# The widest exponential between two upper parts, and weight jobs in quarters

## The reference

```python
scores = np.where(mask, q @ k.T / np.sqrt(64), -1e9)
attn = softmax(scores)                 # row max taken off, sum + 1e-9
x = (attn @ v)                         # to (2304, 512)
h = x @ w_in                           # 512 x 2048
x = (h * np.clip(h + 3, 0, 6) / 6) @ w_out          # first layer
h = x @ w_in2
out = (h * np.tanh(np.log1p(np.exp(h)))) @ w_out2   # second layer
```

## Time and profile before

| what | value |
|---|---|
| median of 3 runs | 994.08 us (991.94 to 994.55) |
| the profiled execution | 992.28 us, with a span of 990.5 us |
| TensorE matmuls busy | 962.7 us (97%) |
| VectorE busy | 758.6 us (77%) |
| ScalarE busy | 644.6 us (65%) |
| GpSimd busy | 446.9 us (45%) |
| mean granted clock | 0.998 of full speed |

### The profile page before, as it was taken

One profiled execution on the slowest core, in us unless ns is written; L12 is line 12 of the kernel. 1 busy time (PEld: TensorE's weight loads), 2 busy tenths in 40 slices (PEclk: granted clock), 3 DMA queues, 4 the chain that ended last, 5 costly groups with the idle time before them and its releaser, 6 DMA issues.

```text
span 990.5 us, 17992 instructions
## 1 busy us (share of the span) xinstructions
PE 962.7 (97%) x6132; PEld 859.8 (87%) x6132; DVE 758.6 (77%) x1443; ACT 644.6 (65%) x1429; POOL 446.9 (45%) x412
## 2 busy tenths in 40 slices
PE   6999899999999999999999999999999999999998
PEld 5888898999888898898889888899889898898896
DVE  5888898978686766769798786876877877777654
ACT  6888788856454554544446556777777777776663
POOL 6776899867765576969676680000000000000000
PEclk9999999999999999999999999999999999999999
DMA  7778667754789978587967545646645645465255
GB/s 163 212 188 253 169 175 203 189 154 145 236 274 326 301 264 285 182 288 273 330 226 259 220 149 177 238 151 219 237 162 211 234 177 196 170 231 201 90 189 194
DMA packets 81914, 211.49 MB, mean 214 GB/s; under 512 B 12320, under 2 KB 19104, under 8 KB 81824
## 3 DMA queue, kind: packets, MB, share of 16 engines
q1 hardware_dynamic: 81744, 210.06, 65.1%
q10 hardware_dynamic: 80, 0.29, 0.1%
HBM read 170.39 MB, written 39.92 MB: 212 GB/s over the span
## 4 chain that ended last, share of the span: by engine, by line
PE 77%; DVE 6%; ACT 2%; DMA 2%; issue 1%; SPq 1%; ACTq 0%; DVEq 0%
PE psum L962 35%; PE psum L845 11%; PE psum L847 11%; PE psum L846 11%; PE psum L795 3%; PE psum L774 3%; PE psum L752 2%; PE psum L754 1%; DVE ebuf L1514 1%; PE psum L750 1%; DVE glo L1520 1%; DVE xlo L1449 1%; DMA ext_d<-ext_made 1%; DMA o_d<-staged 1%; DVE ext_made L1420 1%
## 5 line engine op out<-in xcount | busy, mean ns | idle before, releaser
L962 PE MATMUL psum<-ghi,osplit 128*128 128x512 f32 (+1 forms) x640 | 215.9, 371 | 0.4 <-POOL osplit L1767 0.4
L845 PE MATMUL psum<-xhi,whi 128*128 128x256 f32 (+1 forms) x640 | 187.4, 293 | 2.2 <-ACT snap L1163 2.0
L847 PE MATMUL psum<-xhi,wlo 128*128 128x256 f32 (+1 forms) x640 | 186.8, 292 | 0.0
L846 PE MATMUL psum<-xlo,whi 128*128 128x256 f32 (+1 forms) x640 | 186.6, 292 | 0.0
L962 PE MATMUL psum<-osplit,ghi 128*128 128x512 f32 x576 | 180.9, 395 | 1.1 <-DVE glo L1520 0.9
L1520 DVE SCALAR_TENSOR_TENSOR glo<-ebuf,ghi 128x512 fp32r<-128x512 f32 x144 | 124.0, 861 | 24.8 <-ACT ghi L1211 16.8
L845 PEld LDWEIGHTS psum<-xhi,whi 128*128 128x128 f32 x640 | 120.8, 189 | 15.2 <-ACT snap L1163 3.6
L1767 POOL TENSOR_TENSOR osplit<-oraw,osplit 128x512 fp32r<-128x512 f32 x80 | 115.2, 1442 | 38.4 <-ACT osplit L1130 34.2
L962 PEld LDWEIGHTS psum<-ghi,osplit 128*128 128x128 f32 x640 | 117.9, 189 | 16.4 <-issue 0.6
L1211 ACT ACTIVATE ghi<-ebuf 128x512 fp32r<-128x512 f32 x144 | 90.2, 627 | 62.9 <-DVE ebuf L1514 34.4
L846 PEld LDWEIGHTS psum<-xlo,whi 128*128 128x128 f32 x640 | 120.8, 189 | 10.7
(11 more groups left out here) (113 smaller groups left out, 2250.8 us busy)
## 6 DMA issues: line engine op xcount, KB each, us to landing
ext<-ext_d SPq DMA_DIRECT2D x56, 768.0 KB, 4.3
osplit<-o_d SPq DMA_DIRECT2D x80, 512.0 KB, 5.6
oraw<-in_w_out SPq DMA_DIRECT2D x80, 256.0 KB, 5.6
qkin<-in_qk SPq DMA_DIRECT2D x63, 288.0 KB, 4.4
wraw<-in_w_in SPq DMA_DIRECT2D x32, 512.0 KB, 5.6
ext_d<-ext_made SPq DMA_DIRECT2D x32, 384.0 KB, 5.5
attn_t<-ostage SPq DMA_DIRECT2D x64, 144.0 KB, 3.2
o_d<-staged SPq DMA_DIRECT2D x32, 256.0 KB, 5.2
```

What stands on the lines that cost most here:

```text
L845: pe.matmul(dst, hi, xh, start=(start and cc == 0), stop=False, skip_group_check=True)
L846: pe.matmul(dst, hi, xl, start=False, stop=False, skip_group_check=True)
L847: last = pe.matmul(dst, lo, xh, start=False, stop=(stop and cc == 1), skip_group_check=True)
L962: last = pe.matmul(bank(Y_BANK + c, n), stat, mov, start=(first and m == 0), stop=(final and m == 2), skip_group_check=True)
```

## The change

ScalarE makes the widest exponential between upper parts 0 and 1 instead of behind both. The split of x (steps 21 to 23) moves from the end of ScalarE's step to behind the exponential of tile 1. The first four weight jobs are cut in four pieces of 256 columns, one piece a step: pieces of job m are in ScalarE's steps 1+4m to 4+4m behind the exponential of tile 1, and in VectorE's steps 2+4m to 5+4m behind the second copy. The mixing of job m is in VectorE's step 4m, at the same place, ahead of the piece. The loads of weights move from steps 0, 1, 4, 7, 10, 13 to -1, 3, 7, 11, 15, 19. The counts that others wait for follow from a table, `SPLIT`.

```diff
-EARLY_JOBS = {3: 0, 6: 1, 9: 2, 12: 3}
+QUARTERS, QUARTER_JOBS = 4, 4
+FIRST_QUARTER = [1 + QUARTERS * m for m in range(QUARTER_JOBS)]
-EARLY_LOADS = {0: 0, 1: 1, 4: 2, 7: 3, 10: 4, 13: 5}
+EARLY_LOADS = {-1: 0, 3: 1, 7: 2, 11: 3, 15: 4, 19: 5}
...
+def quarter_at(h):
+
+    for m in range(QUARTER_JOBS):
+        if 0 <= h - FIRST_QUARTER[m] < QUARTERS:
+            return ((m, h - FIRST_QUARTER[m]),)
+    return ()
...
+SPLIT = [sum(QUARTERS if k < QUARTER_JOBS else 1 for k in range(m)) for m in range(len(JOBS) + 1)]
...
                 if m >= 2:
-                    sp.wait_ge(w_lo, m - 1)
+                    sp.wait_ge(w_lo, SPLIT[m - 1])
...
             def attention_step(n):
                 if in_use(n):
                     split_probs_hi(n, 0)
+                    exps(n, 4)
                     split_probs_hi(n, 1)
-                    exps(n, 4)
                 if in_use(n + 3) and n < -1:
                     split_q_hi(n + 3)
                 if in_use(n + 1):
                     exps(n + 1, 0)
-                if in_use(n + 1):
                     exps(n + 1, 1)
+                for m, k in quarter_at(n):
+                    split_quarter_hi(m, k)
+                if n in EARLY_X_HI:
+                    split_x_hi(0, 0, EARLY_X_HI.index(n))
                 if in_use(n):
                     split_probs_hi(n, 3)
...
-                if n in EARLY_X_HI:
-                    split_x_hi(0, 0, EARLY_X_HI.index(n))
-                if n in EARLY_JOBS:
-                    split_res_hi(EARLY_JOBS[n])
+
+            def split_quarter_hi(m, k):
+                act.wait_ge(w_mixed, MIXED[m + 1])
+                cols = slice(k * A_COLS, (k + 1) * A_COLS)
+                nc.scalar.activation(whi[m][:, cols], wraw[m % 2][:, cols], ACT.Copy).then_inc(w_hi, 1)
...
                     copy_o(n, 1)
                     if n % HEADS == HEADS - 1:
                         invert_sums(n // HEADS)
+                if n + 1 in FIRST_QUARTER:
+                    mix_w(FIRST_QUARTER.index(n + 1))
+                for m, k in quarter_at(n - 1):
+                    split_quarter_lo(m, k)
                 if in_use(n + 2):
                     row_max(n + 2, 2)
...
-                if n + 1 in EARLY_JOBS:
-                    mix_w(EARLY_JOBS[n + 1])
-                if n in EARLY_JOBS:
-                    split_res_lo(EARLY_JOBS[n])
...
+            def split_quarter_lo(m, k):
+                dve.wait_ge(w_hi, SPLIT[m] + k + 1)
+                cols = slice(k * A_COLS, (k + 1) * A_COLS)
+                nc.vector.tensor_tensor(wlo[m][:, cols], wraw[m % 2][:, cols], whi[m][:, cols].bitcast(F32),
+                                        ALU.subtract).then_inc(w_lo, 1)
```

More of the change, by code:

```diff
@@ L542, in store_ext_hi @@
                 layer, p = JOBS[m][0:2]
-                sp.wait_ge(w_hi, m + 1)
+                sp.wait_ge(w_hi, SPLIT[m + 1])
                 sp.dma_start(ext_d[layer, p, :, 0:EXT], ext_made[:, 0:EXT].bitcast(F32)).then_inc(ext_hi_stored, 16)
@@ L547, in store_ext_lo @@
                 layer, p = JOBS[m][0:2]
-                sp.wait_ge(w_lo, m + 1)
+                sp.wait_ge(w_lo, SPLIT[m + 1])
                 sp.dma_start(ext_d[layer, p, :, EXT:], ext_made[:, EXT:].bitcast(F32)).then_inc(ext_lo_stored, 16)
@@ L570, in load_ahead @@
                 elif t in (8, 9):
-                    sp.wait_ge(w_lo, 2 * PAIRS - 1 + t % 2)
+                    sp.wait_ge(w_lo, SPLIT[2 * PAIRS - 1 + t % 2])
                 if t >= 2 and t not in (8, 9):
@@ L627, in load_x @@
                         return
-                    sp.wait_ge(w_lo, len(JOBS))
+                    sp.wait_ge(w_lo, SPLIT[len(JOBS)])
                     for i in range(2):
@@ L836, in weights_ready @@
                 if BLOCK_OF[g] % NBL == 0:
-                    pe.wait_ge(w_lo, (3 * PAIRS if layer_of(g) else 0) + p + 1)
+                    pe.wait_ge(w_lo, SPLIT[(3 * PAIRS if layer_of(g) else 0) + p + 1])
             def accumulate(dst, a_hi, a_lo, g, b, n, start, stop):
@@ L1410, in split_res_lo @@
                 p = JOBS[m][1]
-                dve.wait_ge(w_hi, m + 1)
+                dve.wait_ge(w_hi, SPLIT[m + 1])
                 nc.vector.tensor_tensor(wlo[p][:, :], wraw[m % 2][:, :], whi[p][:, :].bitcast(F32), ALU.subtract
                                         ).then_inc(w_lo, 1)
+            def split_quarter_lo(m, k):
[3 more added lines that the diff above has]
+                                        ALU.subtract).then_inc(w_lo, 1)
             def split_ext_lo(m):
                 layer, p = JOBS[m][0:2]
-                dve.wait_ge(w_hi, m + 1)
+                dve.wait_ge(w_hi, SPLIT[m + 1])
                 if layer * PAIRS + p > 0:
```

## The result

The changed kernel took 1009.23 us, median of four runs (1005.41 to 1011.83), beside 993.27 for the kernel before (991.94 to 994.55). The ratio is 1.0158, with a 95% interval of 1.0117 to 1.0199: slower, by 16 us. The forecast was 1002.5, with a range of 994 to 1011. The profiled execution took 1011.1 us, the slower side of its runs, with a span of 1009.3; that of before had 990.5. So the two traces lie 18.8 us apart, where the medians lie 16 apart.

What follows compares the result with a forecast made beforehand. TensorE, busy 97% of 990.5 us, was taken as the bound. Terms: -11.5 - 1.5 + 12.3 + 4.5 + 5.5 = +9.3, giving 1002.5 us as the middle of two bases; range 994 to 1011.

Steps and rivals of the forecast that it cites:

- The late loads: VectorE's four mixings wait for weights that land after the copy; 12.3 us in sum, bounds 0 and 25.
- job 3: Fourth weight job: load issued behind two x chunks, VectorE waits 2.7 us, 3.2 with mix and quarter less slack.
- c: End of VectorE's copy of the second half of a head's attention result; 22.35 us in a clean head.
- The clock: TensorE's granted clock falls to 0.50 behind three of four waits, 1.5 us each; 4.5 us, bounds 0 and 6.
- The old jobs: The four weight jobs' old cost in the heads, x loads among them, vanishes whole; -11.5 us.
- The quarters: VectorE's quarter subtractions collide with GpSimd's q subtraction; thirteen outside mixing heads, ten at 0.5, three at 0.15; 5.5 us.
- My sign of being wrong: Wrong if VectorE shows no wait for the weights, or quarter heads stay at 5.8 to 5.9 us.
- VectorE's gap of 0.19 us: Idle gap on VectorE after its second copy, counted within about 0.2 us of slack in a clean head.
- The exponential: ScalarE's 576-column exponential one upper part earlier helps only where TensorE waits for it; costed at nothing.
- The x heads: Three heads carrying a split of x, which nearly fits ScalarE's idle time, return to 5.80 us; -1.5 us.

Runs made afterwards that it cites:

- early_loads: The changed kernel with its four weight loads moved to steps -2, 1, 5 and 9 (from -1, 3, 7, 11); 992.95 us, ratio 1.0001.
- x_one_later: exp_first with GpSimd's adding and scaling of x one step later and the splits of x in every second step; 987.00 us, ratio 0.9947.
- exp_first: The kernel before with only the widest exponential between upper parts 0 and 1 and the split of x behind tile 1's exponential; 990.97 us, ratio 0.9977.
- early_loads_lo_last: early_loads with VectorE's quarter subtraction moved from ahead of tile 2's row maximum to behind tile 3's; 991.86 us, ratio 0.9997.
- hi_quarters_mix_early: hi_quarters_lo_whole with the mixing one step earlier and the loads at -3, 1, 5, 9; 989.35 us, ratio 0.9975.
- hi_quarters_lo_whole: x_one_later with ScalarE's upper parts of four jobs in quarters, VectorE's lower part whole, loads two steps ahead of the mixing; 991.67 us, ratio 0.9991.

## Why the prediction was right, and where it was off

- **The late loads: right, and the cause.** Moving the four loads back gives the whole 16 us. The waits forecast for VectorE were 1.75, 1.9, 4.3 and 2.7 us; they were 2.53, 2.60, 3.73 and 4.23. Three of the loads landed 4.8 us after issue and that of job 2 3.9, where I had put 4.2. The largest miss is job 3: its load landed after 4.8 us (112.07 to 116.88), and SyncE's step 10 began 0.9 us after c (101.18 against 100.25), as in a clean head, where I had taken 0.4 on the belief that quarters stretch every head. Summed on TensorE I had 12.3 us, and it was 16.2: 2.4 us more wait on VectorE, and 1.5 us more for what stands behind it. What I left out there is that mixing and quarter collide with GpSimd too (1.61 and 0.96 us for the mixings, up to 1.62 for a quarter, where 0.41 is the time alone).
- **The clock: right in kind, half its size.** I took 1.5 us behind three waits, from the one such place in the earlier trace rows. It was 10.3 us behind four. The loss of 1.7 to 3.3 us a wait stands for 3.4 to 6.6 us at 0.50, where the one place before had 3 us, and the clock fell behind the wait of 2.38 us too, for which I had put nothing. This is the term that was mis-sized most: 4.5 against 10.3.
- **The old jobs: 11.5 us, right in sum, in part by luck.** The heads' sum closes with it. But 3.1 us of it are not the jobs': head 15 took 9.96 before, and heads 6 and 12, with the same job work, 6.86; the rest is the wait for the x loads, whose place the change keeps. It all but vanished because GpSimd, held up by the late weights, waited only 0.60 us for x (at 111.18). With the weights early it is back (1.79 us in early_loads), and x_one_later gains by removing it alone (0.9947 against 0.9977 for exp_first). I had let it go with the jobs without a reason.
- **The quarters: right number, wrong reason.** I put 5.5 us on thirteen heads by the collision with GpSimd, 0.5 a head. Measured were 3.8 us. My sign of being wrong, quarter heads of 5.8 to 5.9 us, came for six of the thirteen (5.76 to 5.87), and the others took up to 6.73; the median quarter took 0.42 us, its time alone. The collision is there for some, but early_loads_lo_last shows that TensorE pays about the same without it. I had counted VectorE's gap of 0.19 us as slack that would swallow part of a quarter. In that kernel the gap is still there, 0.19 us, beside heads of 6.06 us: it is a wait for TensorE, and moves with it.
- **The exponential: costed at nothing, worth 2.3 us.** I looked for a wait of TensorE in clean heads and found none, but the old jobs' heads and the x heads had one, and clean heads gained 0.05 as well. In the changed kernel the jobs had left ScalarE's path, so there it should bring the 0.05 a head only; that was argued, not run.
- **The x heads: -1.5 forecast, +0.8 measured for heads 19 to 31.** The split left ScalarE's path, as the working had it, and GpSimd, with 1.28 us more in these steps, was next; 1.06 us is the wait behind the late load of v. I had not asked what is late next.

The x heads (2.3 us too low) and the quarters (1.7 too high) nearly cancel, which is luck; the clock and the longer waits (5.8 + 3.9 us) are the distance between +9.3 and +18.9 in the profiled execution. By the medians it is +16, and 1009.23 us lies near the upper end of the range of 994 to 1011.

## What to carry to other kernels

Before moving a use ahead, work out the distance from its load on the queue's own clock: when the issuing queue reaches the load, how many issues stand before it, and the landing; a table of steps hides that a step on one engine ends where another's is half over. A wait of VectorE cost 1.6 to 1.8 times its length in this kernel (20.9 us for 13.1, and 5.4 for 3.04), so one late load outweighs the whole gain of the moved exponential (2.3). And an operation cut in pieces was free only on the engine with idle time: a piece cost TensorE nothing on ScalarE and 0.31 us on VectorE. Neither form with pieces (989.76 and 989.35 us) beat whole jobs (987.00), but both lost time to a late load of v, so which form is better stays open.

## What the runs showed of the hardware that I had not expected

Four waits of 2.4 to 5.8 us were each followed by 5 to 7 us at a mean granted clock of 0.50 to 0.67; the longest wait did not have the lowest mean, and the loss (1.7, 3.1, 2.2, 3.3 us) does not order with the wait's length. In hi_quarters_mix_early the clock was 0.50 from 107 to 110 behind a wait of 2.09 us, and in hi_quarters_lo_whole it stayed at 1.00 through four waits of 1.4 us. A subtraction on VectorE with both inputs in SBUF took 0.41 us alone and up to 1.65 beside GpSimd's, yet the kernel with the longer ones (median 0.52 us) and the one with the shorter (0.42) took the same time, as far as these runs can tell. The x loads, with the same program up to them, kept GpSimd waiting 4.40 us in one kernel and 3.21 in another, and the head behind them took 11.71 and 8.77 us.
